# A three-stage MoE kernel on one core: moving a small DMA read to the SyncE queue and re-dealing the last ScalarE and VectorE jobs before the down projection

## The reference

```python
attn = linear_attention(q, k, v, w_phi)      # 4 batches, 8 heads, 576 tokens, 64 wide
x = attn as (2304, 512)
# top-1 mixture of 8 experts: every token goes to one expert
h = max(x[mask] @ w1[e], 0); out[mask] = gate * sigmoid * (h @ w2[e])
# dense feed-forward: w_in 512 x 2048, w_out 2048 x 512
h = x @ w_in; g = h * sigmoid(h); return g @ w_out
```

## Time and profile before

| | us |
|---|---|
| median of 3 runs | 905.62 |
| lowest and highest | 902.15 and 912.89 |
| the profiled execution | 905.62 |
| its span in the profile | 903.7 |

### The profile page before, as it was taken

How to read it: one execution, slowest core, us unless ns; L and a number is a source line. 1 busy time by engine, 2 the same in 40 slices (tenths; PEclk the granted TensorE clock), 3 DMA queues, 4 the chain that set the end, 5 groups by cost and what they waited for, 6 DMA issues and landing times.

```text
span 903.7 us, 18947 instructions
## 1 busy us (share of the span) xinstructions
PE 880.0 (97%) x6841; PEld 792.7 (88%) x6842; DVE 552.0 (61%) x822; ACT 431.2 (48%) x794; POOL 298.8 (33%) x265
## 2 busy tenths in 40 slices
PE   7999999978999998999999999999999999999997
PEld 6888888867888886888888889999999999999997
DVE  4767777758801599960090055562468898777882
ACT  4556655651444333433444465664666743333330
POOL 4686776633643455553453200000000011111111
PEclk9999999999999999999999999999999999999999
DMA  5455555416711578734111027645457545344421
GB/s 157 140 154 151 152 154 153 126 35 219 222 52 44 177 240 260 229 106 126 35 61 44 24 68 197 173 126 141 125 177 208 155 155 173 126 129 129 126 85 47
DMA packets 127445, 122.00 MB, mean 135 GB/s; under 512 B 35809, under 2 KB 102497, under 8 KB 127393
## 3 DMA queue, kind: packets, MB, share of 16 engines
q1 hardware_dynamic: 119680, 103.09, 39.3%
q0 software_dynamic: 3504, 11.28, 4.0%
q10 hardware_dynamic: 4208, 6.93, 2.1%
HBM read 86.39 MB, written 34.88 MB: 134 GB/s over the span
## 4 chain that ended last, share of the span: by engine, by line
PE 85%; SPq 4%; DVE 4%; issue 3%; DMA 2%; ACT 0%; POOL 0%; DVEq 0%; POOLq 0%; ACTq 0%
PE bank L712 22%; PE bank L714 22%; PE bank L713 22%; PE bank L786 4%; PE bank L726 3%; PE bank L740 3%; PE bank L913 2%; PE bank L707 2%; DVE w_hi L1526 2%; PE bank L767 2%; SPq L358 1%; PE bank L891 1%; PE bank L760 1%; PE bank L946 1%; SPq L360 1%
## 5 line engine op out<-in xcount | busy, mean ns | idle before, releaser
L695 POOL DMA_INDIRECT out<-temps,ids x18 | 25.1, 1395 | 325.4 <-DVE temps L1555 322.9
L666 POOL TENSOR_TENSOR h_lo<-h_raw,h_hi 128x512 fp32r<-128x512 f32 x49 | 73.1, 1513 | 157.7 <-ACT h_hi L1167 157.7
L712 PE MATMUL bank<-ops,place 128*128 128x384 f32 (+1 forms) x357 | 119.5, 335 | 1.3 <-DVE place L1654 1.1
L714 PE MATMUL bank<-ops,place 128*128 128x384 f32 (+1 forms) x357 | 118.3, 331 | 0.0
L713 PE MATMUL bank<-ops,place 128*128 128x384 f32 (+1 forms) x357 | 118.3, 331 | 0.0
L1617 DVE TENSOR_TENSOR temps<-temps,bank 128x384 f32<-128x384 f32 x72 | 39.8, 553 | 74.9 <-PE bank L714 74.5
L1526 DVE CAST w_hi<-ahead 128x1024 fp32r<-128x1024 f32 x48 | 48.5, 1011 | 56.8 <-PE bank L714 55.6
L712 PE MATMUL bank<-place,ops 128*128 128x256 f32 x294 | 83.2, 283 | 0.0
L713 PE MATMUL bank<-place,ops 128*128 128x256 f32 x294 | 83.2, 283 | 0.0
L714 PE MATMUL bank<-place,ops 128*128 128x256 f32 x294 | 83.2, 283 | 0.0
L712 PE MATMUL bank<-w_hi,xt_hi 128*128 x192 | 78.1, 407 | 2.7 <-DVE w_lo L1528 2.7
(11 more groups left out here) (239 smaller groups left out, 2196.8 us busy)
## 6 DMA issues: line engine op xcount, KB each, us to landing
ahead<-in_moe_w SPq DMA_DIRECT2D x56, 512.0 KB, 4.7
h_rows<-temps SPq DMA_DIRECT2D x96, 192.0 KB, 2.4
w_raw<-h_rows SPq DMA_DIRECT2D x17, 512.0 KB, 4.0
y_sorted<-y ACTq DMA_DIRECT2D x25, 256.5 KB, 2.9
raw<-h_rows SPq DMA_DIRECT2D x10, 512.0 KB, 3.7
tail<-h_rows SPq DMA_DIRECT2D x9, 512.0 KB, 3.7
qk<-in_k SPq DMA_DIRECT2D x32, 128.0 KB, 2.6
vs<-in_v SPq DMA_DIRECT2D x32, 128.0 KB, 2.3
```

Source lines behind the costliest of these rows:

```text
L666: nc.gpsimd.tensor_tensor(h_lo[:, fs, :], h_raw[:, fs, :], h_hi[:, fs, :].bitcast(F32), ALU.subtract).then_inc(h_lo_done, 1)
L712: mm(o, left_hi, right_hi, start=first, stop=False, skip_group_check=shared)
L714: return mm(o, left_lo, right_hi, start=False, stop=last, skip_group_check=shared)
```

## The change

On SP: `load_job(0)` now waits for all of `y_stored` as `load_job(1)` does; `load_job(1)` is issued right behind it, ahead of step 0's stores; and the read of the row numbers moves from POOL to SP, behind both and ahead of step 0's stores. On ACT: `granule_high(0)` moves from step 23 to step 22, ahead of the SiLU of C12 and C21; `granule_high(1)` takes the place of `job_high(10)` in step 23; `job_high(10)`, `granule_high(2)`, `granule_high(3)` and `job_high(11)` follow the last SiLU in this order. On DVE: `job_low(9)` moves from step 22 behind step 23's additions, and `job_sums(11)` and `job_low(11)` move back in the granule loop.

```diff
@@ -466,8 +466,7 @@
 
                 if m < 2:
                     sp.wait_ge(tile_done, T_MAX)
-                    if m:
-                        sp.wait_ge(y_stored, 16 * T_MAX)
+                    sp.wait_ge(y_stored, 16 * T_MAX)
                 else:
                     sp.wait_ge(job_lo, m - 1)
                 if m < NF - U_EARLY:
@@ -510,7 +509,11 @@
                 sp.wait_ge(u_lo, j - U_SLOTS + 1)
                 load_left(u_raw[j - U_SLOTS], j, u_loaded[j - U_SLOTS])
             load_job(0)
-            JOB_AT = {1: 1, 3: 2, 4: 3, 6: 4, 7: 5, 18: 6, 19: 7, 20: 8, 21: 9, 22: 10, 23: 11}
+            load_job(1)
+            with nc.allow_non_contiguous_dma(reason="one number of a row"):
+                sp.dma_start(ids_f[:, :], y_sorted[0:N, D:D + 1].rearrange("(t p) a -> p (t a)", p=P)).then_inc(ids_loaded, 16)
+
+            JOB_AT = {3: 2, 4: 3, 6: 4, 7: 5, 18: 6, 19: 7, 20: 8, 21: 9, 22: 10, 23: 11}
             GRANULE_AT = {17: 0, 18: 1, 19: 2}
             for n in range(STEPS):
                 b, f = divmod(n, NF)
@@ -683,9 +686,6 @@
                     gather(t + 4)
 
 
-            pool.wait_ge(y_stored, 16 * T_MAX)
-            with nc.allow_non_contiguous_dma(reason="one number of a row"):
-                pool.dma_start(ids_f[:, :], y_sorted[0:N, D:D + 1].rearrange("(t p) a -> p (t a)", p=P)).then_inc(ids_loaded, 16)
             pool.wait_ge(ids_loaded, 16)
             step(nc.gpsimd.tensor_copy(ids[:], ids_f[:]))
             for s in range(NS):
@@ -1291,14 +1291,8 @@
                 if edge:
                     op_high(b + 1, M1)
                     op_high(b + 1, M5)
-                if n == STEPS - 1:
-                    granule_high(0)
-                else:
-                    copy_out(n, M5, copy5, ps_c, copied5, C22)
+                copy_out(n, M5, copy5, ps_c, copied5, C22)
                 copy_out(n, M6, copy2, ps_a, copied2, C12)
-                if n == STEPS - 1:
-                    copy_out(n, M5, copy5, ps_c, copied5, C22)
-                    granule_high(1)
                 if n == 0:
                     store_tile(T_MAX - 1, 0)
                 if edge:
@@ -1319,16 +1313,19 @@
                     move_raw(b + 1, 2 * f - 6)
                     move_raw(b + 1, 2 * f - 5)
                 if n == STEPS - 1:
-                    job_high(JOBS - 2)
-                    granule_high(2)
+                    granule_high(1)
+                if n == STEPS - 2:
+                    granule_high(0)
                 silu(n, C12, copy2, v12_done)
                 silu(n, C21, bank[:, ps_a[n % 2], 0:HALF_T], m_done[M4])
 
             for g in range(GRANULES):
                 if g == 0:
+                    job_high(JOBS - 2)
+                if g + 2 < GRANULES:
+                    granule_high(g + 2)
+                if g == 1:
                     job_high(JOBS - 1)
-                elif g + 2 < GRANULES:
-                    granule_high(g + 2)
                 if g % NQ == NQ - 1:
                     copy_acc(g // NQ)
 
@@ -1708,7 +1705,7 @@
                         op_sum(b + 1, i)
                 if 2 <= n < 6:
                     job_low(n - 2)
-                elif STEPS - NF < n < STEPS - 1:
+                elif STEPS - NF < n < STEPS - 2:
                     job_low(n - (STEPS - NF) - 1 + NF - U_EARLY)
                 if 1 <= n < 5:
                     job_sums(n - 1)
@@ -1718,14 +1715,17 @@
                     granule_sums(n - 19)
                 if n == STEPS - 2:
                     granule_low(0)
+            job_low(JOBS - 3)
             granule_low(1)
-            job_low(JOBS - 2)
-            job_sums(JOBS - 1)
             for g in range(GRANULES):
+                if g == 0:
+                    job_low(JOBS - 2)
                 if g + 2 < GRANULES:
                     granule_low(g + 2)
                 if g == 0:
                     granule_sums(3)
+                    job_sums(JOBS - 1)
+                if g == 1:
                     job_low(JOBS - 1)
                 if g + 4 < GRANULES:
                     granule_sums(g + 4)
```

## The result

| | before | after |
|---|---|---|
| median (20 runs each) | 905.55 us | 912.15 us |
| lowest to highest | 902.15 to 912.89 | 908.64 to 917.93 |
| ratio | | 1.0072, 95% interval 1.0049 to 1.0093 |
| the profiled execution, and its span | 905.62, 903.7 | 915.67, 913.8 |

The changed kernel is 0.7% slower, 6.6 us by the medians. That is inside the range I gave and within 1%, but more than twice the 3.1 us of my sum.

The account below looks back on a forecast made before the run. PE was taken as the bound, busy 880.0 of 903.7 us; 2.3 us in step 2 plus 0.8 us at the seam, added to 905.62, gave 908.7 us, counted as no change. Range: 903.5 to 914.0 us.

Parts of the forecast that it names:

- 3.1 us of my sum: Whole kernel: 2.3 us in step 2 plus 0.8 us at the seam, giving 908.7 us, 0.3% slower.
- the hole before M4: PE in step 23: a 0.2 us loss before M4 in the old kernel, predicted to go.
- The 1.0 us of step 23: PE's M6 in step 23: a new 1.0 us stand, as ACT's copy of M1 comes later.
- the wait predicted at granule 4: PE at granule 4: a wait of 0.3 us for DVE's `granule_low(4)`.
- 549.6 + 2.0 + 0.45 against 541.93: Step 2: last store without the read at 549.6, read 2.0 us, SiLU 0.45 us; SP goes on at 541.93.
- the 6.1 us of 300 GB/s: SP's queue: 1.05 MB of jobs in 3.5 us and 0.79 MB of stores in 2.6 us, at 300 GB/s.
- 2.3 + 1.7 - 0.6: The 2.3 is M6 of step 2 predicted late: 0.3 us from queued jobs and stores plus 2.0 us for the read.
- The 2.0 us: SP's queue: the row-number read's delay to step 0's stores, chosen between nothing and 2.9 us.
- the 2.9 us of another transfer's row: SP's queue: at most 2.9 us for the read, scaled by piece count from the `w_head` loads' issue time.
- Rival A: SP's queue: the read is as cheap as its bytes, step 2 stalls 0.3 us; 906.7 us; chance 0.25.
- 3.98 us for the load of granule 3: Granule 3: its load, issued at 721.3 instead of 720.31, lands 3.98 us later, at 725.3.
- the prediction has 0.9: PE at granule 3: a wait of about 0.9 us for `granule_low`.

Follow-up runs that it names:

- seam part: The kernel before with only the change's ScalarE (ACT) and VectorE (DVE) edits, SyncE and POOL as before; measured ratio 1.0018.
- SyncE part: The kernel before with only the change's SyncE edits and without POOL's read, ACT and DVE as before; measured ratio 1.0067.
- read alone ahead: The kernel before with only the read of the row numbers moved to SyncE ahead of step 0's stores, jobs as before; measured ratio 1.0009.
- job 0 alone: The kernel before with only job 0's load also waiting for the last row of y_sorted, ahead of step 0's stores; measured ratio 1.0013.

## Why the prediction was right or wrong

**Right: the places.** PE's idle came exactly where the text had it, in step 2 behind SyncE's queue, in step 23 behind `granule_high(0)` and two SiLUs, and at granule 3; the hole before M4 went. The 1.0 us of step 23 is 1.0 in the change, in the seam part and in every other run with that order. The order of DVE and the issue of granule 3's load, 1 us later relative to PE's work, are as worked out; the wait predicted at granule 4 was swallowed by the longer one at granule 3.

**Wrong, first: the length of SyncE's queue.** By the sum, the copy of M1 of step 2 starts 10.1 us after SyncE goes on (549.6 + 2.0 + 0.45 against 541.93). Measured are 11.8 us, 1.7 us more. Two terms are too small. The read takes 3 us of the queue between the jobs' data and the stores', not 2.0: some 2 us of small pieces, and 1 us of an almost empty queue while SyncE stands inside the issue of the first store, of which I had nothing. And 1.83 MB of jobs and stores at 270 GB/s take 6.8 us, not the 6.1 us of 300 GB/s. That is 1.0 + 0.7 us. What the sum says of ScalarE holds: each SiLU starts as its store lands, and one SiLU and the copy follow the last. Luck hides a part: SyncE went on 0.6 us earlier against PE's work than in the earlier trace rows. So 2.3 + 1.7 - 0.6 = 3.4 us, the measured idle.

The 2.0 us were a choice between nothing and the 2.9 us of another transfer's row, and the latter was nearer. Rival A, a read as cheap as its bytes, is refuted. The run with the read behind the stores shows only 2.0 us less than the changed kernel (9.8 against 11.8; 1.4 less than the run of the SyncE part alone), as it should if the read's pieces still slow its last stores. No run took the read out altogether, so the 3 us are read from the windows of one profile and not confirmed by their absence.

**Wrong, second: the clock was not in the sum.** I priced an idle at its length. After 3.4 us in step 2 and 2.1 us at granule 3 PE ran for some 3.5 us at the lower level, and 3.7 of the 10.1 us between the two spans are this, about 1.8 of the 6.6 us between the medians. Filled with useless matmuls, the same waits cost 2.6 us less. In this stage the profile of before gave no hint, since its only idle, 1.1 us, left the clock alone. In the earlier stages it did: behind a wait of 3.0 us PE's clock was 0.60 from 195 to 199 us.

**Wrong, third: 3.98 us for the load of granule 3.** I took one row as the load's duration. Between executions it went from 4.0 to 5.6 us, and PE's wait went with it, in us:

| | load | PE's wait |
|---|---|---|
| order at the seam as before (before; read alone ahead; job 0 alone; SyncE part) | 4.0, 4.3, 4.4, 5.6 | 1.1, 1.5, 1.6, 2.6 |
| order of the change (read behind the stores; on POOL; the change; seam part) | 4.3, 5.0, 5.2, 5.4 | 1.1, 1.9, 2.1, 2.3 |

In the old order the wait is the load less 2.8 to 3.0 us, in the new one the load less 3.1 to 3.2. So for the same load the new order waits 0.2 to 0.3 us less, not more. With 4.0 us it would wait some 0.8 us, by estimate from these rows, where the prediction has 0.9. So the order was worked out rightly, and the 1.0 us that I booked above for granule 3 is the load's, not the order's. But I had written that the prediction is wrong if PE's waits at granules 3 and 4 exceed 2 us together; at 2.07 us they do, and this is the reason.

**The range.** That 912.15 us lie inside it owes something to its width. It was said to rest on runs of before that differ by up to 7 us; the three shown differ by 10.7.

**What stays open.** What both jobs ahead of the stores cost without the read. By estimate it is 0.4 us of idle (0.3 + 0.7 - 0.6), but that takes a run with no read near them. What decides whether the clock falls after an idle of about two microseconds. And why granule 3's load lands after 4.0 us in one execution and 5.6 in another, and whether the new order has a part in that: its loads are longer in the mean, 5.0 against 4.6 us, but four on each side are too few.

## What to carry to other kernels

A transfer that nobody waits for is not free when it stands in a queue ahead of one that somebody waits for: add up the bytes ahead of the store that frees a buffer, count small pieces apart from bytes, and add what the engine behind that buffer still has to do before the bottleneck gets its operand. Where the clock fell after an idle of the matmul engine (here idles of 1.9 to 3.4 us), it cost from half to nearly all of the idle's length again, so price an idle with what follows, and test by filling it. The mean granted clock of every execution tells whether the profiled one is typical. And a duration read from one row of one profile is a draw: where a wait depends on it, look at its spread before calling the wait a property of the code.

## What the runs showed of the hardware that was not expected

- A SyncE issue is not always 0.37 us. With two jobs of 0.52 MB and 2304 pieces of 4 bytes ahead of it, one store took 4.7 us to issue (4.2 and 4.1 us in the two other runs with that order); behind the jobs alone at most 1.3 us (the run with the read behind the stores), and behind the read alone 1.7 us.
- 2304 pieces of 4 bytes, 9 KB, kept the 16 DMA engines busy for about 2 us, as long as a job of 0.52 MB takes at 270 GB/s (1.9 us). The read landed after 6.3 us on SyncE with jobs ahead and 4.1 us without.
- PE's clock after an idle is not settled by the length alone: it fell after 2.1 us (the changed kernel) and 1.9 us (the read back on POOL), and stayed after 2.3 us (the seam part) and after waits of 1.8 and 1.0 us (the read behind the stores).
- Most of the 10 us between executions of one kernel goes with the mean granted clock: 915.6 to 917.9 us at 0.989 or below, 908.6 to 911.7 us at 0.994 or above (the changed kernel).
